# First layer of dense experts 1 to 7 by Strassen's seven products, in three passes of 1024 tokens

## What is computed

```python
def _moe_ref(x, w_gate, w1, w2):            # N, D, E, F = 3072, 384, 8, 1024
    logits = x @ w_gate
    P = np.exp(logits - logits.max())
    for _ in range(8):
        P /= P.sum(1, keepdims=True) + 1e-09
        P /= P.sum(0, keepdims=True) + 1e-09
        P *= N / E
    for e in range(E):
        h = np.maximum(x @ w1[e], 0.0)
        out += P[:, e:e + 1] * (h @ w2[e])
    return out
def _moe2_ref(x, expert_emb, tau, w1, w2):  # each token goes to its best expert alone
    expert_idx = np.argmax(xn @ en.T / tau, axis=1)
    ...
        h = np.maximum(x[mask] @ w1[e], 0.0)
        out[mask] = gate_w[mask, None] * (h @ w2[e])
```

## Time and profile before

| | |
|---|---|
| median of 3 runs | 2257.34 us (2256.19 to 2260.6) |
| span of the profiled execution, first to last instruction | 2252.6 us |
| its own time with what lies around the span | not listed; the median stands 4.7 us above the span |
| PE busy | 2194.8 us, 97% of the span |
| VectorE busy | 1004.8 us, 45% |
| ScalarE busy | 596.4 us, 26% |
| GpSimd busy | 101.2 us, 4% |
| DMA moved | 175.84 MB, mean 78 GB/s |
| mean granted TensorE clock | 0.984 |
| chain that ended last | PE 91%, DVE 3%, DMA 2%, issue 1% |

### The profile page before, as it was taken

One profiled execution on the slowest core, in us unless ns is written; L12 is line 12 of the kernel. 1 busy time (PEld: TensorE's weight loads), 2 busy tenths in 40 slices (PEclk: granted clock), 3 DMA queues, 4 the chain that ended last, 5 costly groups with the idle time before them and its releaser, 6 DMA issues.

```text
span 2252.6 us, 42581 instructions
## 1 busy us (share of the span) xinstructions
PE 2194.8 (97%) x17887; PEld 2029.6 (90%) x17887; DVE 1004.8 (45%) x1892; ACT 596.4 (26%) x1013; POOL 101.2 (4%) x91
## 2 busy tenths in 40 slices
PE   5899999999999999999999999999999999999998
PEld 5898999999999998999899899989999998899998
DVE  6776556364333232333233232333233335677774
ACT  2423323321111111111111111111111122466664
POOL 0000000000000000000000000000000000122221
PEclk7799999999999999999999999999999999999999
DMA  8645543240000000000000000000000023577662
GB/s 291 207 130 149 143 131 109 83 155 29 1 29 1 29 29 1 29 1 29 1 29 17 13 29 1 29 1 29 1 1 1 1 57 100 178 265 263 236 229 70
DMA packets 154809, 175.84 MB, mean 78 GB/s; under 512 B 81836, under 2 KB 114768, under 8 KB 154642
## 3 DMA queue, kind: packets, MB, share of 16 engines
q1 hardware_dynamic: 143282, 161.58, 22.3%
q0 software_dynamic: 3968, 10.82, 1.3%
q10 hardware_dynamic: 7392, 0.92, 0.3%
HBM read 144.18 MB, written 30.48 MB: 78 GB/s over the span
## 4 chain that ended last, share of the span: by engine, by line
PE 91%; DVE 3%; DMA 2%; issue 1%; SPq 1%; ACT 1%; POOL 0%; ACTq 0%; POOLq 0%; DVEq 0%
PE psA L1896 22%; PE psH L1913 16%; PE psB L1896 9%; PE psB L1913 8%; PE psY L1913 8%; PE psY L2077 5%; PE psH L1789 4%; PE psA L1668 4%; PE psY L1804 4%; PE psA L2063 3%; PE psB L2063 3%; PE psB L1772 1%; DVE products L1168 1%; PE psB L1762 1%; DVE sx L1171 1%
## 5 line engine op out<-in xcount | busy, mean ns | idle before, releaser
L1896 PE MATMUL psA<-X,wh 128*128 128x512 f32 x1440 | 449.3, 393 | 3.0 <-issue 2.2
L1333 DVE SCALAR_TENSOR_TENSOR hl<-psA,hh 128x512 fp32r<-128x512 f32 x240 | 166.1, 692 | 620.7 <-ACT hh L927 620.6
L927 ACT ACTIVATE hh<-psA 128x512 fp32r<-128x512 f32 x240 | 143.8, 599 | 831.9 <-PE psA L1896 831.9
L1896 PEld LDWEIGHTS psA<-X,wh 128*128 128x128 f32 x1440 | 265.9, 188 | 48.7 <-issue 4.6
L1896 PE MATMUL psA<-X,wl 128*128 128x512 f32 x720 | 284.8, 396 | 0.0
L1913 PE MATMUL psH<-wh,hh 128*128 128x384 f32 x672 | 228.4, 340 | 0.0
L1913 PE MATMUL psH<-wh,hl 128*128 128x384 f32 x672 | 227.2, 338 | 0.0
L1913 PE MATMUL psH<-wl,hh 128*128 128x384 f32 x672 | 225.8, 336 | 0.0
L1333 DVE SCALAR_TENSOR_TENSOR hl<-psB,hh 128x512 fp32r<-128x512 f32 x96 | 66.5, 693 | 277.3 <-ACT hh L927 277.2
L1896 PE MATMUL psB<-X,wh 128*128 128x512 f32 x576 | 179.2, 392 | 0.0
L1622 DVE TENSOR_TENSOR vl<-vs,vh 128x768 fp32r<-128x768 f32 x144 | 137.9, 961 | 53.4 <-ACT vh L975 53.2
(11 more groups left out here) (323 smaller groups left out, 4087.9 us busy)
## 6 DMA issues: line engine op xcount, KB each, us to landing
vs<-v_d SPq DMA_DIRECT2D x38, 768.0 KB, 5.8
vs<-v_d SPq DMA_DIRECT2D x19, 1536.0 KB, 11.4
ws<-w_d SPq DMA_DIRECT2D x28, 768.0 KB, 6.1
kT<-kT_d SPq DMA_DIRECT2D x17, 512.0 KB, 5.1
qT<-qT_d SPq DMA_DIRECT2D x15, 512.0 KB, 5.2
a_scratch<-an SPq DMA_DIRECT2D x12, 512.0 KB, 3.8
kq<-kn_d SPq DMA_DIRECT2D x6, 768.0 KB, 5.8
vn<-vn_d SPq DMA_DIRECT2D x12, 384.0 KB, 5.8
```

The costliest lines, as they stand in the source:

```text
L927: act.activation(hh[kk % 3][:, :], ps_h[kk % (2 if last else 3)], ACT.Relu).then_inc(hh_ready, 1)
L1333: dve.scalar_tensor_tensor(hl[b][:, :], ps_h[bank], 0.0, hh[b][:, :].bitcast(F32), ALU.max, ALU.subtract).then_inc(hl_ready, 1)
L1896: mm = pe.matmul(to, a[half][:, c, col], X[:, 2 * g:2 * g + 2, b, c, :], start=(n == 0), stop=(n == 3 * KC - 1))
```

## The change

The 3072 tokens are taken in three passes of 1024 (four chunks of 256), and each pass goes through experts 1 to 7. The unit is a *quad*: 1024 tokens in two groups of 512 by 256 hidden features in two column tiles of 128, with the 384 input features in three chunks. Over the first two chunks the 2 x 2 x 2 block product is formed by Strassen's seven products in Winograd's form, the third chunk adds four plain ones: eleven products of three matmuls. There are 3 x 7 x 4 = 84 quads; each stands for four steps `kk` of before.

- Sums of X (`S1` to `S4`) are made by GpSimd once a pass, and all nine X blocks (`xp`) are split by `spread_high` and `spread_low`. Sums of weights (`T1` to `T4`, `D3`) are made by GpSimd in every quad (`combine`), and the split of first-layer weights then has 1280 columns in place of 768.
- Four products share one bank (`ps_a`). After each of the first three, ScalarE copies the bank to `snap`, and PE goes on adding on it. VectorE adds `ps_c` or `ps_b2` to the copies (`sum_out`); three of the four hidden blocks come from these sums, one from the bank.
- The second layer of a quad (`give`, eight tiles of six matmuls) follows in the next quad. PSUM now collects two feature chunks and not four, so VectorE adds eight tiles per quad.
- X goes to DRAM (`x_dram`) chunk by chunk and is loaded again for each pass; all twelve outputs of expert 0 go through DRAM; the weights of each expert are loaded and split in each pass. The scaling of `acc` by P for expert 0 moves from VectorE to ScalarE (`weigh_y0`).
- Experts 2 onward of a pass are a hardware loop of four quads: six, six and five iterations.
- Eight Sinkhorn halves are left for quads 0 and 1. The turns and scores of a pass's tiles lie in the next pass's first quads; the last eight lie behind the last quad.

```diff
+NPAIR = 3
+PC = NC // NPAIR
+PT = NT // NPAIR
+GT = PT // 2
+TG = GT * P
+QUADS = KF // 2
+PASS = QUADS * (E - 1)
...
+SPREAD = [S1, S2, A11, A22, A12, S4, S3, A13, A23]
+SPREAD_SLOTS = [(0, 0), (0, 4), (4, 7), (7, 9)]
...
+                def load_first_layer(p, e, q):
+
+                    n = quad_of(p, e, q)
+                    if reached(n, 1):
+                        sp.wait_ge(wl1_ready, n)
...
+                    if s - 2 in AT_T:
+                        c = AT_T.index(s - 2)
+                        sp.wait_ge(xf_ready, 2 * c + 1)
+                        sp.dma_start(x_dram[c], xf[:, :, :]).then_inc(x_out, 16)
...
+                sp.wait_ge(y0_out, 16 * PC)
+                load_y0(0)
+                load_first_layer(0, 1, 1)
+                store_y0(NC - 1)
+                sp.wait_ge(y0_out, 16 * 2 * PC)
+                load_y0(1)
+                sp.wait_ge(x_out, 16 * 2 * PC)
+                for k in range(2):
+                    load_source(source, 1, k, k)
+                load_second_layer(0, 1, 1)
+                load_first_layer(0, 1, 2)
...
+                def combine(p, e, q):
+
+                    n = quad_of(p, e, q)
+                    pool.wait_ge(ws1_in, 16 * (n + 1))
+                    pool.tensor_tensor(ws1[:, T1, :], ws1[:, B12, :], ws1[:, B11, :], ALU.subtract).then_inc(combined, 1)
...
+                all_reduce(0)
+                combine(0, 1, 0)
+                for i in range(1, 5):
+                    all_reduce(i)
+                combine(0, 1, 1)
+                all_reduce(5)
+                combine(0, 1, 2)
+                for i in range(6, SINKHORN):
+                    all_reduce(i)
...
+                def high_of_sum(n, par, k):
+
+                    act.wait_ge(t_ready, 3 * n + (1, 2, None, 3)[k])
+                    if reached(n, 2):
+                        act.wait_ge(tile_done, PT * (n - 1))
+                    else:
+                        act.wait_ge(b2_done, NK)
+                        act.wait_ge(y0_out, 16 * NC)
+                    act.activation(hh[par][k][:, :], snap[(0, 2, None, 1)[k]][:, :], ACT.Relu).then_inc(hh_ready, 1)
...
+                    snapshot(n, 0)
+                    snapshot(n, 1)
+                    high_of_sum(n, par, 0)
...
+                    snapshot(n, 2)
+                    high_of_sum(n, par, 1)
...
+                    if not final:
+                        widen_first(n + 1, 1 - par)
+                    widen_second(n, par)
...
+                    high_of_chain(n, par)
...
+                    high_of_sum(n, par, 3)
...
+                def sum_out(n, k):
+
+                    i, ps, others = ((0, ps_c, 1), (2, ps_b2, 3), None, (1, ps_b2, 2))[k]
...
+                    dve.tensor_tensor(snap[i][:, :], ps, snap[i][:, :], ALU.add).then_inc(t_ready, 1)
...
+                    sum_out(n, 0)
...
+                    low_hidden(n, par, 0)
...
+                    sum_out(n, 1)
+                    if given and not (fresh and p == 0):
+                        add(n - 1, p0, e0, 0, fresh)
+                    low_hidden(n, par, 1)
...
+                        add(n - 1, p0, e0, 1, fresh)
...
+                        widen_first(n + 1, 1 - par)
...
+                        add(n - 1, p0, e0, 2, fresh)
+                        add(n - 1, p0, e0, 3, fresh)
+                    widen_second(n, par)
+                    if given and fresh and p == 0:
+                        for t in range(GT):
+                            add(n - 1, p0, e0, t, fresh)
...
+                    low_hidden(n, par, 2)
+                    sum_out(n, 3)
...
+                        add(n - 1, p0, e0, 4, fresh)
+                    low_hidden(n, par, 3)
...
+                        for t in range(GT + 1, PT):
+                            add(n - 1, p0, e0, t, fresh)
...
+                def product(to, p, par, x, w, start, done=None):
+
+                    blocks, weights = xp[p % 2][x], wd1[par]
+                    for n, (a, b) in enumerate(((0, 0), (0, 1), (1, 0))):
+                        mm = pe.matmul(to, weights[:, a, w - 1, :], blocks[:, b, :], start=(start and n == 0), stop=(n == 2), skip_group_check=True)
...
+                def quad(p, e, q, extra=None):
+
+                    n, par = quad_of(p, e, q), q % 2
+                    given = reached(n, 1)
+                    pe.wait_ge(wl1_ready, n + 1)
+                    if given:
+                        pe.wait_ge(hl_ready, 4 * (n - 1) + 3)
+                    product(ps_a, p, par, A11, B11, True, chain_done)
+                    product(ps_c, p, par, A12, B21, True)
+                    product(ps_c, p, par, A13, B31, False, c11_done)
...
+                    pe.wait_ge(snapped, 3 * n + 1)
+                    product(ps_a, p, par, S2, T2, False, chain_done)
+                    if given:
+                        pe.wait_ge(t_ready, 3 * n)
+                    product(ps_b2, p, par, S3, T3, True)
+                    product(ps_b2, p, par, A23, B32, False, second_done)
+                    pe.wait_ge(snapped, 3 * n + 2)
+                    product(ps_a, p, par, S1, T1, False, chain_done)
...
+                        for t in range(GT):
+                            give(n - 1, 1 - par, t)
...
+                    pe.wait_ge(snapped, 3 * n + 3)
+                    product(ps_a, p, par, S4, B22, False)
+                    product(ps_a, p, par, A13, B32, False, chain_done)
...
+                    pe.wait_ge(t_ready, 3 * n + 2)
+                    product(ps_b2, p, par, A22, T4, False)
+                    product(ps_b2, p, par, A23, D3, False, second_done)
+                    if given:
+                        for t in range(GT, PT):
+                            give(n - 1, 1 - par, t)
...
+                for p in range(NPAIR):
+                    pe.wait_ge(xpl_ready, XB * (p + 1))
+                    first_quads(p)
+                    with pe.Fori(2, E if p < NPAIR - 1 else E - 1) as e:
+                        for q in range(QUADS):
+                            quad(p, e, q)
+                last_quads()
```

More of the change, by code:

```diff
@@ L36 @@
 NT = N // P
-TG = 512
-GT = TG // P
-NGRP = N // TG
+NPAIR = 3
[5 more added lines that the diff above has]
+PASS = QUADS * (E - 1)
+NQ = NPAIR * PASS
+QF = 2 * P
+A11, A12, A22, S1, S2, S3, S4, A13, A23 = range(9)
+XB = 9
+SUMS_AT = {S1: 0, S2: 1, S4: 0, S3: 1}
+SPREAD = [S1, S2, A11, A22, A12, S4, S3, A13, A23]
+SPREAD_SLOTS = [(0, 0), (0, 4), (4, 7), (7, 9)]
+B12, B11, B22, B21, B32, B31, T1, T2, T3, T4, D3 = range(11)
+WB = 11
 SINKHORN = 8
@@ L106 @@
 AT_EMB = 22
-SPILLED = 10
+AT_SPREAD = [70 + 2 * j for j in range(XB)]
+AT_COMBINED = 96
 UNITS_ALONE = 2
@@ L637, in load_weights @@
+                with sp.Fori(2, E) as e:
+                    for q in range(QUADS):
+                        load_quad(2, e, q)
                 def load_weights(which, par):
@@ L953, in _ @@
+                for p in range(NPAIR):
+                    first_quads(p)
+                    with act.Fori(2, E if p < NPAIR - 1 else E - 1) as e:
+                        for q in range(QUADS):
+                            quad(p, e, q)
+                for q in range(QUADS):
+                    quad(NPAIR - 1, E - 1, q, final=(q == QUADS - 1))
+                for t in range(NTA, NTA + GT):
+                    squares(t)
+                    take(t)
                 squares(NT - 4)
@@ L1399, in take, with last_adds @@
+                def last_adds():
+                    n = quad_of(NPAIR - 1, E - 1, QUADS - 1)
+                    add(n, NPAIR - 1, E - 1, 0, False)
+                    order_of_big()
+                    for t in range(1, GT):
+                        add(n, NPAIR - 1, E - 1, t, False)
+                    early_rows()
+                    for t in range(GT, PT):
+                        add(n, NPAIR - 1, E - 1, t, False)
+                    take(NT - 3)
+                    take(NT - 1)
                 def take(t):
@@ L1788, in block_hidden @@
                         for a, b in ((wh1, 0), (wh1, 1), (wl1, 0)):
[L1789 removed]
+                            mm = pe.matmul(ps_b[k % 2], a[half][:, c, col], X[u % 2][:, b, c, :], start=(n == 0), stop=(n == 3 * KC - 1))
                             n += 1
```

803 lines of the change are left out of this document (497 added, 306 removed).

## The result

The changed kernel takes 2243.34 us in the median of six runs (2241.22 to 2251.92); beside them on the same chip the kernel before took 2257.19 (2256.19 to 2262.45). The ratio is 0.9942, 95% interval 0.9927 to 0.9958. It is faster, and the time lies in the predicted range, but the gain is 14 us where 32.5 were forecast. The profiled execution has a span of 2240.1 us, 12.5 less than that of before.

A forecast was written before the change was run, and what follows sets the result against it. PE was taken as the bound: number of matmuls times their distance. The terms -58 + 8 + 13 + 1.5 + 2 + 1 gave -32.5 us, so 2225 us, within 2213 to 2236 (63%), outer range 2207 to 2250.

The forecast's parts named there:

- The saving: Dense experts: three first-layer matmuls fewer per quad, 16.06 us a quad, 0.69 saved in each of 84, 58 us in all.
- Loop ends: Ends of hardware-loop iterations in the dense experts: 0.8 us of PE each, fourteen instead of four, costing 8 us more.
- The start: Quads 0 and 1 of the dense experts: PE waits for VectorE, GpSimd and weights; 13 us added, bounds 6 and 22.
- Attention stage: Attention before the dense experts: stores of X delay loads, X splits fit beside PE; 2 us added, between -1 and 8.
- Clock: PE's granted clock behind a pause of 6 us: may drop once, 0 to 3.5 us, taken as 1.5.
- Turns of the passes: First quads of passes 2 and 3: extra X blocks on VectorE, transposed tiles on ScalarE; 1 us, 6 at most.
- The end: Behind the last quad: eight tiles left instead of four; 0 us, between -4 and 4.
- GpSimd beside VectorE: Every quad: SBUF contention costs VectorE up to 2 us, nothing in time because VectorE has 4 us free.
- Rivals 1 and 2: In each quad, GpSimd makes VectorE the bound (2309 us, 5%), or ScalarE's copies come late (2254 to 2284 us, 6%).
- rival 4: Dense start's waits are absorbed and the attention stage is unchanged: about 2213 us, 10%.
- rival 3: Start and seams cost more, with SP's queue, clock and first chunks at upper bounds: +10 to +25, 2236 to 2250 us, 16%.
- the start's three parts: Dense start: PE idle 6 to 7 us before quad 1, 4 inside it, about 2.5 from splitting four X blocks.

The follow-up runs named there:

- e11: The changed kernel with one of its products in every quad (three matmuls of 512 columns) computed and added twice; 2298.29 us, ratio 1.0164.
- e8: The changed kernel with TensorE's loop over experts 2 to 7 of the first two passes given a body of twelve quads instead of four; one run, 2254.74 us.
- e1: The changed kernel with the weight combinations of the first three quads moved from GpSimd to VectorE; 2215.62 us, 0.9803 of the kernel before.
- e2: The kernel of e1 with the four sums of x for the second pass moved to VectorE as well; 2212.56 us, 0.979 of the kernel before.
- e7: The changed kernel with the stores of x of chunks 2 to 11 cut from 128 partitions to one; 2244.03 us, ratio 0.9927.
- e10: The kernel of e2 with the first pass's splits of x moved to other steps; 2207.43 us, 0.9764 of the kernel before.
- e12: The changed kernel with GpSimd's five weight subtractions of every quad done twice; 2261.55 us, ratio 1.0006 to the kernel before.
- e5: The kernel before with a tiny unused GpSimd tensor_tensor behind each of three Sinkhorn all-reduces, plus a small memset; 2287.94 us, ratio 1.0122.
- e9: The kernel before, unchanged, run again for a second profile; one run, 2255.95 us.

## Why the prediction was wrong

The step that failed is the term for the start of the dense experts: it priced GpSimd by its operations and left out what it costs GpSimd to change from one kind to the other. The attention term failed beside it. That the time still lies in the predicted range is luck: the saving and the loop ends came out 10.5 and 11.2 us better than forecast, and with both as forecast the time would have been about 2265 us, slower than the kernel before.

- **The saving**: right, and 0.13 us a quad too small. 84 x (16.748 - 15.933) = 68.5 us instead of 58; e11 shows that PE alone sets the quad. In the trace 48 second-layer matmuls take 8.37 us and not 8.44, and 33 of the first layer 7.56 and not 7.62.
- **Loop ends**: wrong too, in the kernel's favour. I carried the 0.8 us of a body of 48 steps to fourteen ends of a body a third as long; they cost nothing, and the four of before went as well: -3 instead of +8. The Trainium skill (Runtime: NRT & Kernel Launch, "Instruction fetch mechanics") says that a branch to a target outside the instruction window stalls the fetch; that the long bodies pause and the short one does not agrees with it. The evidence here is the four rows of pauses, two of e8 and two of the earlier trace rows.
- **The start**: this is the step that failed. "half 13 waits for an all-reduce that GpSimd does only after `combine` of quad 2" named the right queue, but I priced GpSimd at "0.5 us" around an all-reduce and 2 to 3 us for a combination, from rows in which it never changed between the two kinds. Each change costs 6 to 9. PE idles 33.7 us after the first dense matmul and loses 4.8 to the clock, against 14 and 1.5; and 7.64 us ahead of it, where I had nothing. The turns that e1 takes away cost the kernel 28 us, more than my upper bound of 22 for the whole term. With one turn left (e1) and with none that PE's work waits for (e2), the start idles 17.6 and 11.6 us, about the 14 that I had.
- **Attention stage**: 11.7 us where I had 2 and a bound of 8. The cause I gave, the stores' transfers, has no part in it (e7). 4 to 5 us lie in the last four chunks, with the splits that I costed at nothing; e10 moves the splits and wins 2.8 us there, but the wait that I blamed stays, so their cause is open. The rest is not told apart from what differs between profiles anyway.
- **Clock**: 4.8 us and not 1.5, since the pauses were longer. **Turns of the passes**: 1.16 us of waits, predicted 1. **The end**: less than 1 us, predicted 0. **GpSimd beside VectorE**: nothing in the quad, as said; e12 doubles it and the quad stays. Rivals 1 and 2 are refuted by the loop's window, rival 4 by the start; rival 3's time, 2236 to 2250, is what was measured, for a reason that it did not name and with two terms beside it that went the other way.
- **The sums**: the start's three parts (6 to 7, 4 and 2.5) add up to 12.5 to 13.5 and not 14; rival 4's is 2214.5 and not 2213; rival 3 begins at 2235. None of this changes the outcome.

The sum with the measured terms: -68.5 - 3.2 + 33.7 - 0.85 + 4.8 + 1.2 = -32.9 for the dense stage, measured -30.9; ahead of it 11.7 until the last x and 7.3 from there, where the wait of 7.64 lies, 19.05 us.

## What to carry to other kernels

Before giving an idle engine small work between its other instructions, ask whether it changes kind: on GpSimd a 0.2 us tensor_tensor between two all-reduces took 13 us of its time and 9 of the kernel's, and moving the small work to a busier engine, so that the all-reduces stand in one row, gave 28 us back. A price read from rows where an engine does one thing only bounds nothing for the mix. And when a stage is explained from one trace of each kernel, take a second trace of both first: the waits for kT looked like the change's alone, and shorter ones were in the kernel before too.

## What the runs showed of the hardware

- GpSimd: partition_all_reduce to tensor_tensor 6.9 to 8.9 us of "issue", back 5.8 to 6.1, whether the operation has 2, 128 or 512 columns; none between two of a kind. The Trainium skill (GPSIMD Engine Reference, 2.1 Instruction dispatch) says that the first call of a freshly loaded GpSimd routine pays about 6 us with no instruction to be seen in the profile. The way back, 5.8 to 6.1 us, agrees with it; the way there is a little more. That a turn is such a load isn't shown by these runs. What they show is that it is paid anew at every change and in both directions.
- TensorE pauses 0.4 to 2.7 us at the end of a loop body of about 1000 matmuls and not at one of 324.
- The same attention code reaches x of chunk 7 anywhere in 336 to 344 us in three profiles, with no edit to explain it; e5 and e9, which are 4 us apart, ran on different chips.
